# One weight split a tile, states beside their outputs, and one mask ahead of a fraction

## The chip, the core and the metric

The kernel runs on one core of a Trainium2 chip. Its engines are TensorE (PE, with its weight loads shown as PEld), VectorE (DVE), ScalarE (ACT), GpSimd (POOL) and the DMA queues, most of them fed by SyncE (SP). Each engine works through its own queue in order and waits on semaphores. The metric is the time of one execution in microseconds (us), lower is better.

## The reference, cut to what matters

```python
state = alpha[:, :, t, :, None] * state + einsum('bhd,bhe->bhde', k[:, :, t], v[:, :, t])   # for each of 768 t
y[:, :, t] = einsum('bhd,bhde->bhe', q[:, :, t], state)      # 4 batches, 8 heads, 48 x 48 states
...
x = y as (3072, 384)
h = x @ w_in; g = h * cos(h); x = g @ w_out                  # 384 -> 2048 -> 384
h = maximum(maximum(x @ w1, x @ w2), x @ w3); out = h @ w_out2   # 384 -> 768 -> 384
```

All in fp32. A decayed linear attention, then a cosine-gated layer, then a layer with a maximum of three products.

## The kernel before

**Precision.** A matrix product in fp32 is made of three in fp32r: each operand is split into a high part (a copy by ACT) and a low part (operand minus high part, by DVE or POOL), and `split_mm` issues high*high, low*high and high*low (L1293 to L1295).

**Stages.** The 768 steps of time are cut into 6 chunks of 128 tokens (x 4 batches = 512 columns). The attention of a chunk is 16 units (a pair of heads in one batch). The first layer's 2048 hidden features are 16 tiles of 128; in general, tile `i` of chunk `c` runs beside unit `i` of the attention of chunk `c + 1`. Chunk 0 has nobody to run beside, so its layer is cut in two half steps of 256 columns. The first half step, on which everything here turns, does tiles 0 to 15 for the first two batches while the units 8 to 15 of chunk 0 are still being done. Only units 0 to 7 stand ahead of it. The second half step (tiles counted on as 16 to 31) does the other two batches beside the attention of chunk 1.

**One tile of the first half step.** PE: `hidden1(i)` (9 matmuls into one of three banks in turn), then `accumulate1(i - 3)` (9 matmuls), then, for tiles in `SCORE_AT` (5 to 9, 11 to 13), `stage1` of a unit (scores and transposed keys), and, for tiles in `OUTPUT_AT` (6 to 9, 11 to 14), `outputs` and `increment` of the unit whose scores were made in a tile before. Units 8 to 15 alternate between two score banks: `stage1(0, u)` waits until the mask of unit `u - 1` is done and until the state of unit `u - 2` has been copied out of the bank. ACT: `turn(i)` (h in turns), `rounded(i)`, `g_high(i - 1)`, `cosines(i)`. DVE: `fraction(i)` between `rounded` and `cosines`, then `gate(i)`. POOL: `g_low(i)`, for which `accumulate1(i)` waits. So one tile's chain is hidden, turn, round, fraction, cosine, gate, high part, low part, accumulate.

**Other work laid between them by hand.** ACT also copies the high parts of the first layer's weights (`high_weights(k)`, one 128x768 copy a tile of weights, called "high k" below), the units' first states (`first_state(u)`, two 48x48 copies), splits of the keys and of x. The low parts of the weights (`low_weights(k)`, "low k") are made by DVE for k = 5, 8, 9, 10, 11 (table `low0`) and by POOL for the others (three pieces of 256 columns each). `hidden1(k)` waits for low k. DVE further does the masks of scores (`mask_scores`, waited for by `outputs`), the scan of the decays, its reciprocals (`inverse`), and POOL the products with the decays (`mul_decay`, `mul_inverse`). The order of each engine is what the program text says: there is no scheduler. `x_high0(3)` and `x_low0(3)`, in tile 15, split the last part of the second half step's x.

Of the kernel before, what the change touches and what calls it, by code (L numbers as in the profile page):

```python
# [17 lines left out]
UNITS = PAIRS * BATCH  # L18
TILES1 = FF1 // P
# [32 lines left out]
SCORE_AT = dict(zip((5, 6, 7, 8, 9, 11, 12, 13), range(FIRST_UNITS, UNITS)))  # L52
OUTPUT_AT = dict(zip((6, 7, 8, 9, 11, 12, 13, 14), range(FIRST_UNITS, UNITS)))
# [15 lines left out]
def build(nc, qka, val, wa, wb, spill, out):  # L69
# [8 lines left out]
    with ctx:  # L78
# [454 lines left out]
        def _(act):  # L533
# [20 lines left out]
            def high_weights(k):  # L554
                at = slice(k * W1COLS, (k + 1) * W1COLS)
                act.wait_ge(S[f"stage_in{k % SLOTS1}"], 16 * (k // SLOTS1 + 1))
                nc.scalar.activation(w_hi[:, at], stage[k % SLOTS1], ACT.Copy).then_inc(S["whi_done"], 1)

            def first_state(u):

                p, b = place0(u)
                act.wait_ge(S["inc_done"], u + 1)
                for row, col in ((0, 0), (64, HD)):
                    rr, cc = slice(row, row + HD), slice(col, col + HD)
                    nc.scalar.activation(state[rr, p * BATCH + b, cc], banks(u)[1][rr, cc],
                                         ACT.Copy).then_inc(S["state_done"], 1)
# [98 lines left out]
            for i in range(TILES1):  # L665
                last = i == TILES1 - 1
                if i == 10:
                    x_high0(2)
                if last:
                    x_high0(3)  # L670
                if i - 1 in OUTPUT_AT and not last:
                    first_state(OUTPUT_AT[i - 1])
                turn(i, True)
                if i == 1:
                    g_high(0, True)
                rounded(i)
                if i > 4:
                    g_high(i - 1, True)
                if i in (3, 8, 14):
                    split_keys(*{3: (0, 2), 8: (0, 3), 14: (1, 0)}[i])  # L680
                cosines(i, True)
                if 0 < i < 5:
                    high_weights(4 + i)
                if i in (1, 2, 3):
                    g_high(i, True)
                if 3 < i and 5 + i < TILES1:
                    high_weights(5 + i)
            g_high(TILES1 - 1, True)
            first_state(UNITS - 1)

            def split_high(t, s, part):

# [146 lines left out]
        def _(dve):  # L839
# [168 lines left out]
            ahead0 = {**{i: (0, 2, 2 + i) for i in range(2)}, **{i + 3: (0, 3, i) for i in range(4)},  # L1008
                      **{i + 8: (1, 0, i) for i in range(4)}, **{i + 13: (1, 1, i) for i in range(3)}}
            scan0 = {8: (1, 0), 10: (1, 1)}  # L1010
            low0 = {1: (5,), 5: (8,), 6: (9,), 7: (10, 11)}
            for i in range(TILES1):
                if i == 10:
                    x_low0(2)
                if i == TILES1 - 1:
                    x_low0(3)
                fraction(i, True)
                if i in scan0:
                    scan(*scan0[i])
                if i in SCORE_AT:  # L1020
                    mask_scores(0, SCORE_AT[i])
                early = i and i not in scan0 and i not in SCORE_AT
                if i in ahead0 and early:
                    inverse(*ahead0[i], ahead0[i][0] % 2)
                gate(i, True)
                if i == 2:
                    scan(0, 3)
                if i in ahead0 and not early:
                    inverse(*ahead0[i], ahead0[i][0] % 2)
                for k in low0.get(i, ()):  # L1030
                    low_weights(k)
# [523 lines left out]
```

## Time and profile before

| what | value |
|---|---|
| time, median of 3 runs | 842.2 us (842.09 to 842.33) |
| the profiled execution: its own time | 843.79 us |
| the profiled execution: its span, first to last instruction | 842.1 us |
| mean granted TensorE clock | 0.998 |
| PE busy in the span | 823.2 us (98%) |
| DVE, ACT, POOL busy | 582.0, 428.0, 245.7 us |
| first half step, from PE's first `hidden1` to the first of the next half step | 24.6 to 73.2 us of the span |

In the trace, times are counted from the span's start. A line of a timeline has start, duration, engine, line, operation, output and inputs, and in brackets how long the engine sat idle before it and for what. Matmuls overlap each other: what counts for PE is the distance from start to start. Also on ACT, DVE and POOL a successor's start lies some 0.1 us before the recorded end of the one ahead.

### The profile page before, as it was taken

The numbers are of one execution on the slowest core, as the hardware profiler recorded it, in microseconds if no ns is written. First come the engines' busy times: TensorE is split into PE (matmuls) and PEld (weight loads), VectorE is DVE, ScalarE is ACT, GpSimd is POOL, SyncE is SP. The second block draws the span as 40 slices with busy tenths as digits, with TensorE's granted clock in tenths as the row PEclk, the third lists the DMA queues.
The fourth block names the chain that finished last, engine by engine and source line by source line (L and its number), as shares of the span: only waits on it lengthen the run. The fifth ranks groups of instructions, "written<-read, shape, count | busy, mean of one in ns | idle before, by whom it ended". The sixth has DMA issues, their size and how long they took to land.

```text
span 842.1 us, 15514 instructions
## 1 busy us (share of the span) xinstructions
PE 823.2 (98%) x5446; PEld 757.6 (90%) x5446; DVE 582.0 (69%) x1080; ACT 428.0 (51%) x933; POOL 245.7 (29%) x272
## 2 busy tenths in 40 slices
PE   5899999999999999999999999999999999999998
PEld 5789998888888888888888888899999999999998
DVE  7797776877687767776874477676664655665554
ACT  4887775444554454445544456554343534334333
POOL 7886673444244425432442133200000000000000
PEclk9999999999999999999999999999999999999999
DMA  8832432322042204211312002210111010100001
GB/s 240 262 110 62 110 78 74 87 58 58 29 123 57 58 29 122 59 52 35 94 67 76 7 35 72 94 57 1 39 39 38 39 39 37 37 35 3 1 39 38
DMA packets 13778, 54.48 MB, mean 65 GB/s; under 512 B 1968, under 2 KB 2480, under 8 KB 13712
## 3 DMA queue, kind: packets, MB, share of 16 engines
q1 hardware_dynamic: 12992, 49.70, 20.6%
q0 software_dynamic: 720, 3.93, 1.2%
q8 instruction: 38, 0.62, 0.3%
q14 instruction: 28, 0.23, 0.1%
HBM read 44.19 MB, written 9.44 MB: 64 GB/s over the span
## 4 chain that ended last, share of the span: by engine, by line
PE 95%; DVE 2%; ACT 2%; issue 1%; ACTq 0%; DVEq 0%
PE h_ps L1293 7%; PE h_ps L1295 7%; PE h_ps L1294 7%; PE acc_pair L1293 5%; PE acc_pair L1294 5%; PE acc_pair L1295 5%; PE h_ps L1399 4%; PE score L1399 4%; PE h_ps L1401 4%; PE h_ps L1400 4%; PE score L1401 4%; PE score L1400 4%; PE acc_last L1293 3%; PE acc_last L1295 3%; PE acc_last L1294 3%; PE score L1257 3%
## 5 line engine op out<-in xcount | busy, mean ns | idle before, releaser
L463 POOL TENSOR_TENSOR work<-work 128x512 f32<-128x512 f32 (+1 forms) x90 | 119.5, 1328 | 278.8 <-DVE work L993 261.6
L635 ACT ACTIVATE work<-work 128x512 f32<-128x512 f32 (+1 forms) x112 | 63.7, 569 | 136.6 <-POOL work L463 123.0
L1293 PE MATMUL h_ps<-x_hi,w_hi 128*128 128x512 f32 (+1 forms) x282 | 111.3, 395 | 1.8 <-DVE x_lo L929 1.5
L979 DVE TENSOR_TENSOR work<-work,h_ps 128x512 f32<-128x512 f32 (+1 forms) x94 | 58.6, 623 | 67.3 <-ACT work L635 66.6
L1295 PE MATMUL h_ps<-x_lo,w_hi 128*128 128x512 f32 (+1 forms) x282 | 104.3, 370 | 0.0
L1294 PE MATMUL h_ps<-x_hi,w_lo 128*128 128x512 f32 (+1 forms) x282 | 103.5, 367 | 0.0
L871 DVE RECIPROCAL inv_decay<-decay 112x128 f32<-112x128 f32 x96 | 89.6, 942 | 0.5
L642 ACT ACTIVATE g_hi<-work 128x512 fp32r<-128x512 f32 (+1 forms) x112 | 63.5, 567 | 43.0 <-DVE work L979 41.7
L1293 PE MATMUL acc_pair<-g_hi,w_hi 128*128 128x512 f32 (+1 forms) x224 | 81.7, 365 | 0.1
L1295 PE MATMUL acc_pair<-g_lo,w_hi 128*128 128x512 f32 (+1 forms) x224 | 80.4, 359 | 0.0
L1294 PE MATMUL acc_pair<-g_hi,w_lo 128*128 128x512 f32 (+1 forms) x224 | 80.4, 359 | 0.0
L528 POOL DMA_DIRECT2D out<-raw x5 | 2.9, 575 | 258.9 <-DVE raw L1182 258.9
L985 DVE TENSOR_TENSOR g_lo<-work,g_hi 128x512 fp32r<-128x512 f32 x80 | 61.1, 764 | 14.9 <-ACT g_hi L642 13.6
L615 ACT ACTIVATE work<-h_ps 128x512 f32<-128x512 f32 (+1 forms) x83 | 46.8, 564 | 30.7 <-PE h_ps L1295 29.6
L1295 PEld LDWEIGHTS h_ps<-x_lo,w_hi 128*128 128x128 f32 x282 | 53.6, 190 | 9.6
L1293 PEld LDWEIGHTS h_ps<-x_hi,w_hi 128*128 128x128 f32 x282 | 53.9, 191 | 9.1 <-issue 1.8
L1399 PE MATMUL h_ps<-x_hi,w_hi 128*128 128x256 f32 x216 | 61.7, 286 | 0.0
L1399 PE MATMUL score<-x_hi,w_hi 128*128 128x256 f32 x216 | 61.7, 286 | 0.0
L1400 PE MATMUL score<-x_hi,w_lo 128*128 128x256 f32 x216 | 61.1, 283 | 0.0
L1400 PE MATMUL h_ps<-x_hi,w_lo 128*128 128x256 f32 x216 | 61.1, 283 | 0.0
L1401 PE MATMUL h_ps<-x_lo,w_hi 128*128 128x256 f32 x216 | 60.8, 282 | 0.0
L1401 PE MATMUL score<-x_lo,w_hi 128*128 128x256 f32 x216 | 60.8, 282 | 0.0
(232 smaller groups left out, 2402.2 us busy)
## 6 DMA issues: line engine op xcount, KB each, us to landing
v_all<-val SPq DMA_DIRECT2D x24, 576.0 KB, 3.7
raw<-qka SPq DMA_DIRECT2D x46, 291.0 KB, 4.6
block_out<-x SPq DMA_DIRECT2D x6, 768.0 KB, 6.0
x_in<-block_out SPq DMA_DIRECT2D x6, 768.0 KB, 4.3
raw<-wb SPq DMA_DIRECT2D x12, 384.0 KB, 3.2
out<-raw POOLq DMA_DIRECT2D x5, 768.0 KB, 3.5
stage_own<-wa SPq DMA_DIRECT2D x6, 384.0 KB, 7.7
x<-wa SPq DMA_DIRECT2D x6, 384.0 KB, 7.0
```

The lines of the kernel that those rows point to most:

```text
L463: nc.gpsimd.tensor_tensor(frac[:, cols], turns[:, cols], whole[:, cols], ALU.subtract).then_inc(S["frac_done"], 1)
L635: nc.scalar.activation(cosine[:, cols], frac[:, cols], ACT.Sin, scale=-TURN if half and t < POOL_FRAC else TURN).then_inc(S["cos_done"], 1)
L642: nc.scalar.activation(g_hi[:, odd, at], gated[:, cols], ACT.Copy).then_inc(S["ghi_done"], 1)
L871: nc.vector.reciprocal(inv_decay[R, s, b].rearrange("d (h n) -> d h n", h=2), decay[R, s, b].rearrange("d (h n) -> d h n", h=2)[:, :, D_LO ...
L979: nc.vector.tensor_tensor(gated[:, cols], cosine[:, cols], h, ALU.mult).then_inc(S["g_done"], 1)
L985: nc.vector.tensor_tensor(g_lo[:, odd, at], gated[:, cols], g_hi[:, odd, at].bitcast(fp32), ALU.subtract).then_inc(S["glo_done"], 1)
L1293: mm(ps, w_hi[:, w_at], xh, start=first, stop=False, skip_group_check=shared)
L1294: mm(ps, w_lo[:, w_at], xh, start=False, stop=False, skip_group_check=shared)
L1295: return mm(ps, w_hi[:, w_at], xl, start=False, stop=final, skip_group_check=shared)
L1399: mm(ps, hi, x_h, start=start, stop=False, skip_group_check=grown)
L1400: mm(ps, lo, x_h, start=False, stop=False, skip_group_check=grown)
L1401: return mm(ps, hi, x_l, start=False, stop=stop, skip_group_check=grown)
```

## The change

Three edits of the first half step, and no instruction is added or taken out.

1. ACT's `high_weights` stand one a tile: high 5 to 15 in tiles 1 to 11. Before, tile 4 had high 8 and high 9, and tiles 5 to 10 had high 10 to 15. High 9 to 15 thus move one tile later.
2. ACT's `first_state(u)` stands in the tile of the unit's outputs, behind `cosines(i)` and ahead of the weights; before, it stood at the head of the next tile (that of unit 15 at the end of the half step; it now stands in tile 14, ahead of `x_high0(3)`).
3. DVE: the mask of unit 8 stands ahead of `fraction(5)` and no longer behind it. Low 8 moves from tile 5 to 6, low 9 from 6 to 7, low 10 stays in 7, and low 11 moves from 7 to 9.

```diff
@@ ACT, loop over the tiles of the first half step
                 if last:
                     x_high0(3)
-                if i - 1 in OUTPUT_AT and not last:
-                    first_state(OUTPUT_AT[i - 1])
                 turn(i, True)
...
                 cosines(i, True)
-                if 0 < i < 5:
+                if i in OUTPUT_AT:
+                    first_state(OUTPUT_AT[i])
+                if 0 < i < TILES1 - 4:
                     high_weights(4 + i)
                 if i in (1, 2, 3):
                     g_high(i, True)
-                if 3 < i and 5 + i < TILES1:
-                    high_weights(5 + i)
             g_high(TILES1 - 1, True)
-            first_state(UNITS - 1)
@@ DVE, loop over the tiles of the first half step
-            low0 = {1: (5,), 5: (8,), 6: (9,), 7: (10, 11)}
+            low0 = {1: (5,), 6: (8,), 7: (9, 10), 9: (11,)}
...
+                if i == 5:
+                    mask_scores(0, SCORE_AT[i])
                 fraction(i, True)
                 if i in scan0:
                     scan(*scan0[i])
-                if i in SCORE_AT:
+                if i in SCORE_AT and i != 5:
                     mask_scores(0, SCORE_AT[i])
```

ACT in the tiles 4 (from its cosine) to 6. L557 is `high_weights`, L615 `turn`, L623 `rounded`, L642 `g_high`, L635 `cosines`, L565 `first_state`; x2 and x2_in are staging slots, high 8 and 9 come from x2, high 10 and 11 from x2_in. Before:

```order
L635 ACTIVATE work<-work 128x256
L557 ACTIVATE w_hi<-x2 128x768 x2
L615 ACTIVATE acc_last<-acc_last 128x256
L623 ACTIVATE work<-acc_last 128x256
L642 ACTIVATE g_hi<-work 128x256
L635 ACTIVATE work<-work 128x256
L557 ACTIVATE w_hi<-x2_in 128x768
L615 ACTIVATE h_ps0<-h_ps0 128x256
L623 ACTIVATE work<-h_ps0 128x256
L642 ACTIVATE g_hi<-work 128x256
L635 ACTIVATE work<-work 128x256
L557 ACTIVATE w_hi<-x2_in 128x768
```

The same place after:

```order
L635 ACTIVATE work<-work 128x256
L557 ACTIVATE w_hi<-x2 128x768
L615 ACTIVATE acc_last<-acc_last 128x256
L623 ACTIVATE work<-acc_last 128x256
L642 ACTIVATE g_hi<-work 128x256
L635 ACTIVATE work<-work 128x256
L557 ACTIVATE w_hi<-x2 128x768
L615 ACTIVATE h_ps0<-h_ps0 128x256
L623 ACTIVATE work<-h_ps0 128x256
L642 ACTIVATE g_hi<-work 128x256
L635 ACTIVATE work<-work 128x256
L565 ACTIVATE state<-score0 48x48 x2
```

One copy of weights (high 9) has moved behind tile 5's cosine, high 10 behind tile 6's, and the state of unit 8 stands straight behind tile 6's cosine.

DVE from `gate(4)` on. Before, L1002 is `fraction`, L892 `mask_scores`, L979 `gate`, L871 `inverse`, L940 `low_weights`, L861 `scan` (each number is 3 less in the changed file). Before, tiles 4 to 6:

```order
L979 TENSOR_TENSOR work<-work,h_ps1 128x256
L1002 SCALAR_TENSOR_TENSOR work<-work,acc_last 128x256
L892 TENSOR_TENSOR scores<-score0,mask 128x304
L979 TENSOR_TENSOR work<-work,acc_last 128x256
L871 RECIPROCAL inv_decay<-decay 112x128
L940 TENSOR_TENSOR w_lo<-x2,w_hi 128x768
L1002 SCALAR_TENSOR_TENSOR work<-work,h_ps0 128x256
L892 TENSOR_TENSOR scores<-score1,mask 128x304
L979 TENSOR_TENSOR work<-work,h_ps0 128x256
L871 RECIPROCAL inv_decay<-decay 112x128
```

The same place after:

```order
L976 TENSOR_TENSOR work<-work,h_ps1 128x256
L889 TENSOR_TENSOR scores<-score0,mask 128x304
L999 SCALAR_TENSOR_TENSOR work<-work,acc_last 128x256
L976 TENSOR_TENSOR work<-work,acc_last 128x256
L868 RECIPROCAL inv_decay<-decay 112x128
L999 SCALAR_TENSOR_TENSOR work<-work,h_ps0 128x256
L889 TENSOR_TENSOR scores<-score1,mask 128x304
L976 TENSOR_TENSOR work<-work,h_ps0 128x256
L868 RECIPROCAL inv_decay<-decay 112x128
L881 COPY from_mid<-decay 112x2x2
L937 TENSOR_TENSOR w_lo<-x2,w_hi 128x768
```

The first mask has passed the fraction, and low 8 stands behind the reciprocal of tile 6 and no longer behind that of tile 5.

DVE once more, in the changed kernel, from the scan of tile 8 to the next scan, in tile 10:

```order
L858 SCALAR_TENSOR_TENSOR decay<-raw,starts 112x528
L889 TENSOR_TENSOR scores<-score1,mask 128x304
L976 TENSOR_TENSOR work<-work,acc_last 128x256
L868 RECIPROCAL inv_decay<-decay 112x128
L999 SCALAR_TENSOR_TENSOR work<-work,h_ps0 128x256
L889 TENSOR_TENSOR scores<-score0,mask 128x304
L976 TENSOR_TENSOR work<-work,h_ps0 128x256
L868 RECIPROCAL inv_decay<-decay 112x128
L937 TENSOR_TENSOR w_lo<-x2_in,w_hi 128x768
L921 TENSOR_TENSOR x_lo0<-y_ps,x_hi 96x2x256
L999 SCALAR_TENSOR_TENSOR work<-work,h_ps1 128x256
L858 SCALAR_TENSOR_TENSOR decay<-raw,starts 112x528
```

Low 11 (L937) is what is new in this stretch, at the end of tile 9.

## Rows read from the trace of the kernel before

**Rows 1.** Busy of PE, PEld, DVE, ACT, POOL by stretch; clock, DMA share, GB/s.

```profile
40.00:80.00 40.00, 36.93 (x320) 36.10 (x318) 33.15 (x63) 32.01 (x88) 29.02 (x38) 1.00 0.33 91
80.00:842.00 762.00, 757.81 (x4940) 694.49 (x4938) 517.34 (x962) 370.68 (x786) 185.57 (x184) 1.00 0.18 53
```

**Rows 2.** Waits of PE, 38 to 70 us, longest: total, times, longest one.

```profile
PE y_ps L1272 <- DVE scores L892: 1.9, 1, 1.9
```

**Rows 3.** Timeline of PE: hidden or accumulate of tiles, scores, outputs.

```profile
42.62 0.43 PE L1272 MATMUL y_ps<-scores,v_all 128*96 128x128 f32 x2 [1.93 <-DVE scores L892]
...
46.65 0.46 PE L1257 MATMUL score<-q_dec,k_split 112*128 112x128 f32 x2 [1.07 <-ACT state L565]
...
47.75 0.36 PE L1293 MATMUL acc_last<-x_hi,w_hi 128*128 128x256 f32 x1
...
56.73 0.28 PE L1293 MATMUL acc_last<-x_hi,w_hi 128*128 128x256 f32 x1
...
61.06 0.28 PE L1293 MATMUL acc_pair<-g_hi,w_hi 128*128 128x256 f32 x1
...
62.02 0.28 PE L1295 MATMUL acc_pair<-g_lo,w_hi 128*128 128x256 f32 x1
62.37 0.46 PE L1257 MATMUL score<-q_dec,k_split 112*128 112x128 f32 x2
...
74.38 0.28 PE L1293 MATMUL acc_pair<-g_hi,w_hi 128*128 128x256 f32 x1
...
75.61 0.46 PE L1257 MATMUL score<-q_dec,k_split 112*128 112x128 f32 x2
```

**Rows 4.** Timeline of ACT: tiles 4, 5, 6, the key split of 8, and 15.

```profile
39.39 1.56 ACT L557 ACTIVATE w_hi<-x 128x768 fp32r<-128x768 f32 x2
40.86 0.36 ACT L615 ACTIVATE acc_last<-acc_last 128x256 f32<-128x256 f32 x1
...
42.13 0.42 ACT L635 ACTIVATE work<-work 128x256 f32<-128x256 f32 x1 [0.18 <-DVE work L1002]
42.45 0.83 ACT L557 ACTIVATE w_hi<-x_in 128x768 fp32r<-128x768 f32 x1
...
46.09 0.42 ACT L565 ACTIVATE state<-score 48x48 f32<-48x48 f32 x2
...
50.50 1.25 ACT L589 ACTIVATE k_split<-k_dec 64x512 f32<-64x512 f32 x2
```

**Rows 5.** Timeline of DVE: tiles 4 to 8, and the scan of tile 10.

```profile
39.81 0.36 DVE L979 TENSOR_TENSOR work<-work,h_ps 128x256 f32<-128x256 f32 x1
...
42.01 0.47 DVE L892 TENSOR_TENSOR scores<-score,mask 128x304 f32<-128x304 f32 x1
...
45.82 0.95 DVE L871 RECIPROCAL inv_decay<-decay 112x128 f32<-112x128 f32 x1
...
46.70 0.95 DVE L940 TENSOR_TENSOR w_lo<-x,w_hi 128x768 fp32r<-128x768 f32 x1
...
48.80 2.38 DVE L940 TENSOR_TENSOR w_lo<-x_in,w_hi 128x768 fp32r<-128x768 f32 x2
...
51.43 1.46 DVE L861 TENSOR_TENSOR_SCAN decay<-raw,starts 112x528 f32<-112x528 f32 x1
...
57.89 2.10 DVE L861 TENSOR_TENSOR_SCAN decay<-raw,starts 112x528 f32<-112x528 f32 x1
```

**Rows 6.** Timeline of POOL: low weights, low parts of g (g_lo), tiles 7 to 14.

```profile
50.68 1.10 POOL L471 TENSOR_TENSOR g_lo<-work,g_hi 128x256 fp32r<-128x256 f32 x1 [0.32 <-ACT g_hi L642]
51.73 3.06 POOL L453 TENSOR_TENSOR w_lo<-stage_own,w_hi 128x256 fp32r<-128x256 f32 x3
...
55.45 2.14 POOL L453 TENSOR_TENSOR w_lo<-stage_own,w_hi 128x256 fp32r<-128x256 f32 x3
...
58.83 1.69 POOL L471 TENSOR_TENSOR g_lo<-work,g_hi 128x256 fp32r<-128x256 f32 x1
...
73.42 0.73 POOL L471 TENSOR_TENSOR g_lo<-work,g_hi 128x256 fp32r<-128x256 f32 x1 [3.44 <-ACT g_hi L642]
```

## The prediction, made before the changed kernel was run

> **What bounds the kernel now.** I read the busy time by stretch first. Behind 80 us PE is busy for 757.81 of 762.00 us at full granted clock, with DVE at 517 and ACT at 371 [rows 1]: from there on the time is PE's own work, so what PE gains or loses ahead of that point arrives at the end unchanged. Of the 40 us before it PE is busy for 36.93: 3.07 us are missing [rows 1]. The view of PE's waits, read next, says where: 1.9 us for the mask of unit 8 [rows 2]. PE's timeline has it as the gap that ends at 42.62, and beside it one of 1.07 that ends at 46.65, for the state of unit 8 [rows 3]: together 3.0. Nothing else of that size exists, so 3.1 us (0.4%) is about the most that this change can give. Whether it gives them depends on the chains of ACT, DVE and POOL, read last.
>
> **Part 1: the two waits.** Both come from tile 4's double weight copy. The two copies start at 39.39 and the turn of tile 5 at 40.86 [rows 4], so a copy costs 0.73 from start to start. From a turn to the cosine, through round and fraction, it is 42.13 - 40.86 = 1.27, and from the cosine to the next instruction 0.32 [rows 4]. A pair of states takes 0.44 (0.42 and the usual distance).
> With one copy, turn 5 starts at 40.12, cosine 5 at 41.39, high 9 at 41.71, turn 6 at 42.44, cosine 6 at 43.71, the state of unit 8 at 44.03. The score that waits for this state started 46.65 - 46.09 = 0.56 behind it [rows 3, 4], so now 44.6.
> The mask: gate 4 ends at 39.81 + 0.36 = 40.17 [rows 5] and is touched by nothing in the change, the mask follows at 40.2, and the output came 42.62 - 42.01 = 0.61 behind it [rows 3, 5]: 40.8, in place of 42.62. ACT and DVE are both free for this, and the unit's scores are older. The fraction that the mask now precedes waits for ACT until 40.9, so the mask's 0.47 costs nothing there.
> Then PE does tile 7's hidden and waits for accumulate 4 (its g_lo stands behind POOL's old work, about 0.3), then for the score at 44.6, and has its output of unit 9 done at 45.7, where before the next hidden started at 47.75 [rows 3]. So far 2.05 us are won.
>
> **Part 2: low 8 becomes late.** Hidden 8 needs low 8, which has moved behind the reciprocal of tile 6. Gate 6 starts when cosine 6 has ended (0.42 [rows 4]), at 44.15, the reciprocal at 44.5. From reciprocal to low weights it is 46.70 - 45.82 = 0.88, and the subtraction takes 0.95 [rows 5]: low 8 runs from 45.36 to 46.3. Hidden 8 starts at 46.4 and not at 45.7. Of 2.05 us 1.35 are left.
>
> **Part 3: the stretch of tiles 7 to 11.** Fraction 7 stands behind low 8 (46.2), so cosine 7 is at 46.65. Add 0.32, the states 0.44, high 11 0.73: turn 8 at 48.15. Turn, round and g_hi take 1.0 until the key split, which takes 1.28 (two of 1.25 together [rows 4]): cosine 8 at 50.4, states, high 12 at 51.2, turn 9 at 51.9, so ACT's tile 9 could have its cosine at 53.2.
> DVE does low 9 and low 10 from 47.4. A pair took 2.38, where one alone takes 0.95: the POOL subtraction beside it took 1.10 in place of 0.73 [rows 5, 6]. These are two engines blocking each other, and I take the pair's time: fraction 8 at 49.8. The scan of tile 8 took 1.46 with the same kind of neighbour [rows 5]; mask 11 is at 51.6, gate 8 at 51.9, then reciprocal (0.33 + 0.87), fraction 9 at 53.1, cosine 9 at 53.6, state 0.44, high 13 from 54.35 to 55.2. Gate 9 follows at 54.05, the reciprocal, and low 11 from 55.25 to 56.2. Hidden 11 waits for it: 56.3, in place of 56.73 [rows 3]. Left: 0.4 us.
>
> **Part 4: POOL, the term that decides.** Before, POOL worked without a break from 51.73 (low 12) to 58.83 + 1.69 = 60.52 (g_lo of tile 9) [rows 6], and accumulate 9 started at 61.06 [rows 3]: a margin of 0.5 us only. Now low 13 cannot start before high 13 is there, at 55.2, where before it started at 55.45 [rows 6], right behind its predecessor. From there POOL has the three pieces (2.14 - 0.05), two products with decays (58.83 - 55.45 - 2.1 = 1.3) and the g_lo (0.73), 4.1 us. On top come the blocks. The scan of tile 10 cost the g_lo of tile 9 1.69 - 0.73 = 0.96 before; it does so again, since it moves to about 57.1 and into POOL's busy stretch. New is low 11, which starts at 55.25 beside low 13: a block of 0.4 (the g_lo at 50.68) to 0.96: 1.10 and 1.69 against 0.73 [rows 6]. Low 12 gained the like (3.06 before for what takes 2.14 [rows 6]), but that gain is lost, as POOL waits for high 13. Together 55.2 + 4.1 + 1.9 = 61.2; with 0.4 for low 11 it is 60.7. I take the upper one, as two instructions start within 0.1 us of each other and the whole subtraction lies in the way. Accumulate 9 then starts at 61.25, 0.2 later than before.
> On what this block is: the row shows a POOL subtraction stretched from 0.73 to 1.69 beside a DVE scan [rows 5, 6]. The Trainium skill (SBUF — State Buffer, section Who interferes with whom) says that a DVE instruction with two SBUF inputs and a GpSimd instruction that reads SBUF exclude each other for a whole instruction. The trace agrees. By that rule the block of low 11 is 0.95 less what has already run, so the sum would be the 61.2 above; by the mildest row it would be 60.7.
>
> **Part 5: what remains.** The score of tile 12 had a gap ahead of it: it starts 0.35 behind the previous matmul, where 0.12 is usual (62.02, 62.37) [rows 3]. It waited for a state copied at the head of tile 12, which now comes in tile 11, at 61.3 or earlier: -0.2. In tile 14, the states of unit 15 now stand ahead of x_high0(3), so g_hi 14 and with it g_lo 14 come 0.44 later against PE. The g_lo ends at 73.42 + 0.73 = 74.15 and accumulate 14 starts at 74.38 [rows 3, 6], margin 0.2: +0.25. The score at 75.61 waited for that same state (its 0.46 in place of 0.39 shows a restart), and no longer does: -0.2. The start of the second half step on x_low0(3) has some 0.7 us to spare. DMA: the loads of weights behind low 8 and low 9 are issued up to 1.7 us later, and are used more than 5 us behind that: nothing.
>
> **Sum.** +0.2 (accumulate 9) + 0.1 (restart) - 0.2 + 0.25 - 0.2 = +0.15 us against the span of 842.1, so 842.25. The profiled execution took 843.79 in all, 1.7 above its span, but the median of the plain runs is 842.2; the difference is carried over to that: 842.35, and I write 842.3. A measurement of this kernel can tell 0.2% (1.7 us) from no change; the forecast is no change.
>
> **Rivals.**
> *The gain survives (chance 0.30).* If low 9 and 10 take 1.7 in place of 2.38, high 13 and low 11 come 0.5 earlier, POOL is less blocked and accumulate 9 starts at 60.6 or before. Then part 2's and 3's rests stay: 0.5 to 1.2 us, so 841.4. For it: one DVE subtraction beside a POOL one took 0.95 only [rows 5]. Against: the pair of the very same shape took 2.38.
> *The two waits go and nothing takes their place (0.05).* 3.1 us less the 0.25 above and some bubble: 840.0 or up to 840.5. Against it stand two due times, low 8 at 46.3 and low 11 at 56.2, that follow from rows of DVE without any block.
> *Slower: low 11 loses the port (0.15).* If POOL's first piece of low 13 starts ahead of low 11, and the second too, low 11 ends at 57.3: hidden 11 starts 0.6 later than before, POOL's chain is pushed as well, and part 5 is added: 843.0. It decides once low 11 ends behind 56.6. The scan at 57.89 that took 2.10 and not 1.46 [rows 5] shows that DVE can lose twice.
> *The forecast (0.50).* Two waits of 3.0 us go, and waits for low 8, low 11, g_lo 9 and g_lo 14 come in their place.
>
> **Range and chances.** The forecast alone spans 841.9 to 842.7 (the block of low 11 between 0.4 and 0.96). With the surviving gain down to 841.2, and the slower case up to 842.9, at most 2 in 10 are left out. Faster by over 0.2% needs the case without new waits: 0.05. Slower by over 0.2% would need three lost turns in a row: 0.03. Within 0.2%: 0.92.
>
> **What would show it.** Right: the output at 40.8 and the score at 44.6 in PE's timeline; a wait of PE for low weights of DVE ahead of hidden 8 (0.7) and ahead of hidden 11; a wait for POOL's g_lo at accumulate 9; low 13 of POOL starting with an idle gap for ACT. Wrong: PE running without a gap from 46 to 61 (then the gain stays), or accumulate 9 with a margin; low 9 and low 10 in under 1.9 together; any new wait behind 80 us, of which this reckoning has none.

## The result and the profile after

The changed kernel takes 846.78 us (median of 5 runs, 844.61 to 847.26). The kernel before, run beside it, takes 842.2 (842.09 to 842.78). The ratio is 1.0047, with a 95% interval of 1.0032 to 1.0062: slower by about 4 us (the two medians are 4.6 apart), where I had forecast no change and a range of 841.2 to 842.9.

The profiled execution of the changed kernel took 845.47 us in all, with a span of 843.8. Busy time by stretch (PE, PEld, DVE, ACT, POOL, each with its count; clock, DMA share, GB/s), the rows that answer to [rows 1]:

```profile
40.00:80.00 40.00, 34.70 (x292) 33.44 (x293) 34.17 (x59) 29.70 (x80) 27.21 (x35) 1.00 0.33 90
80.00:842.00 762.00, 759.66 (x4960) 696.63 (x4958) 518.90 (x963) 372.34 (x791) 186.57 (x186) 1.00 0.17 53
```

PE lacks 5.3 us of the 40 where it lacked 3.07 before [rows 1]; behind 80 us it is as dense as ever. So the loss lies where the change was made. This execution has only a part of it: from the cosine of tile 4 to the end of its span it takes 843.8 - 38.4 = 805.4 us, and the kernel before 842.1 - 39.1 = 803.0. The other part is worked out at the end of the experiments. The waits of PE from 22 to 90 us (total, times, longest one) answer to [rows 2]:

```profile
PE score L1256 <- ACT state L565: 2.6, 2, 2.2
PE h_ps L1292 <- DVE x_lo L926: 1.5, 1, 1.5
PE acc_last L1292 <- DVE w_lo L937: 1.4, 2, 0.8
PE acc_pair L1292 <- POOL g_lo L471: 1.2, 2, 0.9
```

The 1.9 for the mask is gone. The forecast waits are there: low weights of DVE (1.4), g_lo (1.2), a short one for a state (0.4). One is in no step of the prediction: 2.2 us for a state. PE's timeline, answering to [rows 3], has it at 67.74, ahead of the score of tile 13:

```profile
43.91 0.46 PE L1256 MATMUL score<-q_dec,k_split 112*128 112x128 f32 x2 [0.43 <-ACT state L565]
...
45.78 0.36 PE L1292 MATMUL acc_last<-x_hi,w_hi 128*128 128x256 f32 x1 [0.56 <-DVE w_lo L937]
...
55.51 0.36 PE L1292 MATMUL acc_last<-x_hi,w_hi 128*128 128x256 f32 x1 [0.84 <-DVE w_lo L937]
...
61.00 0.38 PE L1292 MATMUL acc_pair<-g_hi,w_hi 128*128 128x256 f32 x1 [0.94 <-POOL g_lo L471]
...
67.74 0.46 PE L1256 MATMUL score<-q_dec,k_split 112*128 112x128 f32 x2 [2.16 <-ACT state L565]
```

The whole trace lies 0.7 us earlier than that of before (cosine 4 at 38.36 and not 39.07). That is no work of the change: in the traces of all kernels below, whose program is the same up to there, this cosine lies anywhere from 37.60 to 39.10. So 0.7 must be added to compare with rows of before.

Who held the state? ACT's timeline: it waited 4.88 us for DVE's fraction of tile 12, and copied the state of unit 13 behind its cosine.

```profile
66.86 0.42 ACT L635 ACTIVATE work<-work 128x256 f32<-128x256 f32 x1 [4.88 <-DVE work L999]
67.18 0.42 ACT L565 ACTIVATE state<-score 48x48 f32<-48x48 f32 x2
```

And DVE's timeline, answering to [rows 5]:

```profile
61.08 0.42 DVE L976 TENSOR_TENSOR work<-work,acc_last 128x256 f32<-128x256 f32 x1 [1.49 <-POOL g_lo L471]
61.42 0.94 DVE L868 RECIPROCAL inv_decay<-decay 112x128 f32<-112x128 f32 x1
62.28 3.53 DVE L874 TENSOR_TENSOR to_mid<-decay,from_mid 112x4 f32<-112x4 f32 x1
65.74 0.76 DVE L881 COPY from_mid<-decay 112x4 f32<-112x4 f32 x1
66.42 0.41 DVE L999 SCALAR_TENSOR_TENSOR work<-work,h_ps 128x256 f32<-128x256 f32 x1
```

A product of four columns took 3.53 us, and the copy of four columns behind it 0.76. In the kernel before the same two, which I call the pair, took

```profile
63.13 0.54 DVE L877 TENSOR_TENSOR to_mid<-decay,from_mid 112x4 f32<-112x4 f32 x1
63.59 0.16 DVE L884 COPY from_mid<-decay 112x4 f32<-112x4 f32 x1
```

POOL's timeline of the changed kernel, answering to [rows 6]:

```profile
60.22 1.43 POOL L471 TENSOR_TENSOR g_lo<-work,g_hi 128x256 fp32r<-128x256 f32 x2
61.60 2.12 POOL L453 TENSOR_TENSOR w_lo<-x,w_hi 128x256 fp32r<-128x256 f32 x3
63.67 0.73 POOL L471 TENSOR_TENSOR g_lo<-work,g_hi 128x256 fp32r<-128x256 f32 x1
64.37 2.11 POOL L453 TENSOR_TENSOR w_lo<-x,w_hi 128x256 fp32r<-128x256 f32 x3
```

POOL's subtractions run back to back at their undisturbed 0.7 us while the product is pending, and end at about 62.3, 63.0, 63.7, 64.4, 65.1 and 65.8. The product was issued at 62.28 and ended with the last of these: DVE let four or five ends pass. Before, it got in as soon as the subtraction that was running had ended (63.13 to 63.67).

### The profile page after: what moved, and what is told of

Read it like the earlier page. It is cut to its first block, busy times and chain, and to the rows that moved or that the text cites. A ratio compares the mean times of both kernels' runs of the same rounds, so it can differ in the third digit from the quotient of the medians.

```text
span 843.8 us, 15514 instructions
## 1 busy us (share of the span) xinstructions
PE 821.8 (97%) x5446; PEld 755.3 (90%) x5446; DVE 585.4 (69%) x1080; ACT 427.7 (51%) x933; POOL 245.5 (29%) x272
## 4 chain that ended last, share of the span: by engine, by line
PE 91%; ACT 2%; DVE 2%; issue 2%; POOL 2%; DMA 0%; ACTq 0%; POOLq 0%; DVEq 0%
PE h_ps L1292 7%; PE h_ps L1294 6%; PE h_ps L1293 6%; PE acc_pair L1292 5%; PE acc_pair L1293 5%; PE acc_pair L1294 5%; PE h_ps L1398 4%; PE score L1398 4%; PE h_ps L1400 4%; PE h_ps L1399 4%; PE score L1400 4%; PE score L1399 4%; PE acc_last L1292 3%; PE acc_last L1293 3%; PE acc_last L1294 3%; PE y_ps L1275 2%
## 5 line engine op out<-in xcount | busy, mean ns | idle before, releaser
L635 ACT ACTIVATE work<-work 128x512 f32<-128x512 f32 (+1 forms) x112 | 63.7, 569 | 139.8 <-POOL work L463 122.9
L642 ACT ACTIVATE g_hi<-work 128x512 fp32r<-128x512 f32 (+1 forms) x112 | 63.5, 567 | 42.7 <-DVE work L976 41.4
L615 ACT ACTIVATE work<-h_ps 128x512 f32<-128x512 f32 (+1 forms) x83 | 46.7, 562 | 30.8 <-PE h_ps L1294 29.7
```

Source lines behind the costliest of these rows:

```text
L635: nc.scalar.activation(cosine[:, cols], frac[:, cols], ACT.Sin, scale=-TURN if half and t < POOL_FRAC else TURN).then_inc(S["cos_done"], 1)
L642: nc.scalar.activation(g_hi[:, odd, at], gated[:, cols], ACT.Copy).then_inc(S["ghi_done"], 1)
```

## The experiments

Seventeen kernels ran. Each is compared with runs of the kernel before on the same chip, whose median was between 842.55 and 843.11. "Changed" and "before" say which kernel an edit starts from.

**Is the pair the loss?** First, in the changed kernel, a reciprocal of one input from SBUF in place of the product. This leaves the product out in tile 11, so the output is another and only the time is read:

```diff
+ if a == 1 and p == 0:
+     dve.wait_ge(S["inv_done"], BATCH * g + BATCH)
+     nc.vector.reciprocal(to_mid[R, s], inv_decay[R, s, :, HALF - 1])
+ else:
      nc.vector.tensor_tensor(to_mid[R, s], decay[R, s, :, HALF], from_mid[R, 1 - odd, p], ALU.mult)
```

> The changed kernel, but in tile 11 the product for to_mid (112x4, two inputs in SBUF, 3.53 us in the trace after) is a reciprocal of one input: the product is left out there, so the output differs and only the time is read. Theory A (this tiny instruction loses the shared SBUF port to POOL's unbroken run of subtractions again and again; all the rest is as forecast): 842.3 +- 0.4 us, with runs within 0.7 us of each other, and the tile's instructions take under 0.3 us. Rival B (the loss is the late high weights and POOL's chain to g_lo 9, and to_mid only shows it): stays at 844.5 to 847.

Measured 844.64 (844.17 to 849.67, 11 runs), ratio 1.0031 [1.0020, 1.0043]. A miss, and a telling one. DVE's timeline:

```profile
61.77 0.18 DVE L876 RECIPROCAL to_mid<-inv_decay 112x4 f32<-112x4 f32 x1
61.86 3.26 DVE L885 COPY from_mid<-decay 112x4 f32<-112x4 f32 x1
```

The one-input reciprocal got in at once (0.18), and the stall moved to the copy. So a second input from SBUF is not needed for it. Next the pair as a whole goes to tile 15, in the changed kernel and in the kernel before:

```diff
-                if b == BATCH - 1:
+                if b == BATCH - 1 and not (a == 1 and p == 0):
...
+                if i == TILES1 - 1:
+                    middle(1, 0, 1)          # product and copy
```

> The changed kernel with the whole computation, but the two tiny instructions behind the last reciprocal of that group (product to_mid and copy from_mid) moved from tile 11 to tile 15, where POOL is idle. Theory A: 842.3 +- 0.4 us with a narrow spread, and the product takes 0.1 us. Rival B: 844.5 to 847 as before.

> The kernel before, with only the tiny product and copy moved from tile 11 to tile 15 (whole computation). In the trace of before they took 0.54 and 0.16 us in tile 11, DVE was not what PE waited for there. Theory A (in before the pair got in at the first gap, by the phase of POOL's stream): 842.3 +- 0.4, no change. Rival C (before too loses to POOL in some executions, which its median hides): lower median by up to 0.5 and a narrower spread than the 841.9 to 843.7 of before.

The changed kernel without the pair in tile 11 takes 842.97 (842.62 to 844.23, 11 runs), ratio 1.0005 [0.9996, 1.0014]. Its product takes 0.10 and its copy 0.15, and PE's waits from 38 to 90 us are

```profile
PE acc_last L1300 <- DVE w_lo L943: 1.4, 2, 0.9
PE acc_pair L1300 <- POOL g_lo L471: 1.2, 2, 0.9
PE score L1264 <- ACT state L565: 0.4, 1, 0.4
```

These are the waits of the forecast: 3.0 us in place of 3.0 us. The kernel before with the same edit takes 843.05 (ratio 1.0005 [0.9996, 1.0014]): it lost nothing by the pair. So the pair's place in the changed schedule is the whole loss of 4 us, and the rest of the change is worth nothing that these runs can tell.

**Which half of the change brings it?** ACT's part alone (the diff's edits 1 and 2) and DVE's part alone (edit 3):

```diff
# ACT alone: in the changed kernel, DVE as before (the mask of unit 8 too, left out here)
-            low0 = {1: (5,), 6: (8,), 7: (9, 10), 9: (11,)}
+            low0 = {1: (5,), 5: (8,), 6: (9,), 7: (10, 11)}
# DVE alone: in the changed kernel, ACT as before (the states too, left out here)
-                if 0 < i < TILES1 - 4:
+                if 0 < i < 5:
                     high_weights(4 + i)
+                if 3 < i and 5 + i < TILES1:
+                    high_weights(5 + i)
```

> The kernel before with ACT's part of the change alone (one weight a tile, states in the tile of their outputs); DVE's order is that of before. High 13 is late for POOL as in the changed kernel, so POOL runs unbroken up to tile 11's tiny product. Theory A: slower with a wide spread, 843 to 847, if the product lies in POOL's unbroken run in its trace, with over 1 us for it. Rival B: 844 to 847 with a short product. If neither: low 11 in tile 7 waits for high 11 and costs DVE about 0.8 us, 842.5.

> The kernel before with DVE's part alone (mask of unit 8 ahead of the fraction of tile 5, low 8, 9 and 11 later); ACT's order is that of before, so high 12 and 13 are early for POOL. Theory A: the time goes by whether the tiny product meets an unbroken POOL: 841.5 to 842.5 and narrow if it takes under 0.7 us, up to 846 if not. Rival B (late high weights are the loss): 841.2 to 842.3, whatever the product takes.

ACT's part alone: 845.69 (845.3 to 846.0, 5 runs), ratio 1.0035 [1.0022, 1.0048]. DVE's part alone: 846.11 (845.75 to 846.4), ratio 1.004 [1.0027, 1.0053]. Either half brings the stall, on the copy in the one (3.54 us) and on the product in the other (3.53).

```profile
60.73 0.77 DVE L874 TENSOR_TENSOR to_mid<-decay,from_mid 112x4 f32<-112x4 f32 x1
61.42 3.54 DVE L881 COPY from_mid<-decay 112x4 f32<-112x4 f32 x1
```

Those two rows are of ACT's part alone. The moved mask by itself, from the kernel before (`mask_scores` of tile 5 ahead of `fraction(5)`, nothing else):

> The kernel before with only the mask of unit 8 moved ahead of the fraction of tile 5. By the steps of the prediction fraction 5 does not wait for the mask, and the output of unit 8 comes about 0.7 us earlier (fraction 5 starts at 41.7 as before, the mask at 40.2 in its idle time): PE then waits longer for the state of unit 8 at 46.65 (0.4 earlier), so 0.3 to 0.6 us are gained if nothing else moves: 841.9. Theory A: if the tiny product meets POOL's unbroken run in its trace with 3 us, it is 844 to 846 instead, in spite of the smaller wait.

843.29 (843.05 to 843.54), ratio 1.0008 [0.9999, 1.0017]; expected was a gain. PE's longest wait shows why there is little: the 1.9 for the mask became a longer one for the state, which ACT still copied in the next tile. PE waits 2.5 us in place of 3.0, and that half us doesn't show in the time.

```profile
PE score L1259 <- ACT state L565: 2.5, 1, 2.5
```

**Does the rest of the forecast leave something to win?** The pair in tile 15, and low 8 and low 11 ahead of their reciprocals:

```diff
+                if i in (6, 9):
+                    for k in low0.get(i, ()):
+                        low_weights(k)
```

> The changed kernel with product and copy in tile 15 (as in the run at 842.97) and, besides, low 8 and low 11 ahead of the reciprocals of tiles 6 and 9. Whole computation. By the prediction's own steps the waits of PE for low 8 (0.8) and low 11 (0.8 in the trace) go; PE then waits for g_lo 9 until about the same time as now, since POOL's chain hangs on high 13. So if POOL's chain is what bounds (prediction, part 4), the gain over the run at 842.97 is 0 to 0.4 us: 842.6 to 843.0. If low 8 and low 11 were what binds, it is 0.8 or more: 842.1 or less.

842.9 (842.42 to 844.03), ratio 1.0006 [0.9997, 1.0015]. PE's wait for DVE's low weights fell from 1.4 to 0.9 (that for low 8 is gone, that for low 11 stays) and the one for g_lo from 1.2 to 1.0; no time clear of the noise came of it. Which chain bounds next isn't shown, and no version beat the kernel before.

**Why does DVE lose so many turns?** Two probes put a test stretch behind the whole kernel before: POOL subtracts 128x256 blocks without a pause, and DVE issues tiny products and copies between reciprocals; in the second, at 28 positions against POOL's instruction, twice over for the products and twice for the copies, once each beside a POOL that waits for a semaphore after every third subtraction. PE and ACT have nothing to do in these stretches, unlike in the kernel.

```diff
+            for n in range(96):                       # POOL
+                last = piece_of(n)
+            for n in range(28):                       # DVE
+                filler(96 + 4 * n)                    # a reciprocal of growing width
+                nc.vector.tensor_tensor(to, decay[R, 0, :, HALF], from_mid[R, 0, 0], ALU.mult)
```

> The kernel before, with a test stretch behind its end that measures the disputed cost by itself: POOL runs 150 subtractions 128x256 back to back, beside it DVE runs reciprocals 112x128 with, between them, 10 tiny products (112x4, two SBUF inputs), 10 tiny copies (112x4) and 4 subtractions 128x384; then POOL runs bursts of three with a pause, beside 9 more tiny products. Theory A: in the unbroken stream some or all tiny products and copies take 2.8 to 3.6 us (four or five POOL instructions), the reciprocals 0.94 throughout, and in the bursts no product takes over 1.5 us. Rival D (a tiny instruction waits for the POOL instruction that runs, and gets in at its end): none takes over 0.8 us, and the 3.5 us of the changed kernel have another cause.

> The kernel before with another test stretch behind its end. In the first probe all tiny instructions waited 0.5 us, but each arrived at the same point of POOL's instruction, since the last wait had set the phase. Now the reciprocal ahead of each has another width (96 to 204 columns), so that 28 tiny products and then 28 tiny copies arrive at points spread over POOL's 0.69 us; each once beside a stream of POOL without semaphores and once beside one in groups of three with a semaphore, as its low weights are. Theory E (a tiny instruction that arrives in the last few hundredths of a us of a POOL instruction loses several turns in a row): most take 0.1 to 0.8 us, and one or two of each sweep 2.8 to 3.6. Rival D (it always gets in at the next end of a POOL instruction): all under 0.8. Rival F (a stream in which POOL's next instruction waits for nothing never lets go for 3 us): over 2.8 us at all phases beside the first stream and not beside the second.

The first gave 0.50 to 0.59 for every tiny instruction, the second these (duration min/median/max in ns):

```profile
L1278 DVE TENSOR_TENSOR v_all<-decay,from_mid x56: 91/336/627, 848.6 to 948.8; 112x4 f32<-112x4 f32 x56
L1280 DVE COPY v_all<-decay x56: 98/344/633, 979.8 to 1080.1; 112x4 f32<-112x4 f32 x56
```

None waited longer than one POOL subtraction takes. So neither a long unbroken stream of POOL nor the phase of the request is enough by itself. The phase was then tried in the real place, by a reciprocal of 48 or 60 columns ahead of the pair:

```diff
+                        if a == 1 and p == 0:
+                            nc.vector.reciprocal(idle[R, 0:48], decay[R, s, 0, 1:49])   # 60 in the kernel before
```

> The changed kernel with one reciprocal of 48 columns (0.36 us, one input) ahead of the product for to_mid in tile 11, so that it arrives in the middle of a POOL instruction and not 0.02 us ahead of its end. Theory E (phase): the product takes under 0.8 us, time 842.5 to 843.5. Rival G (any place in that stretch of POOL loses until the third piece of low 15): the product still takes 3.1 us, time 844.5 to 847.

> The kernel before with one reciprocal of 60 columns (0.44 us) ahead of the product for to_mid in tile 11, so that it arrives 0.04 us ahead of the end of a POOL instruction instead of 0.48. Theory E (phase): the product or the copy takes about 3 us, time 844 to 846. Rival G: in at the next end, 0.1 to 0.8 us, time 842.5 to 843.

The changed kernel stays at 847.26 (846.51 to 847.66), ratio 1.0054 [1.0037, 1.0070], with a product of 3.21 us; the kernel before stays at 843.09, ratio 1.0001 [0.9991, 1.0011], with a product of 0.15. The phase is out.

**Is it POOL's semaphores?** My next theory, H in the expectations, was that DVE gets in where a wait of POOL was met shortly before. In the kernel before, the g_hi for which POOL's g_lo of tile 11 waits ended at 63.34, just ahead of the end at which DVE got in. So I gave the changed kernel a wait at that place that is met just as shortly before, and as its control the same wait met long before; and I let the kernel before go on, behind low 14, with low 15, whose inputs are long there.

```diff
# fresh wait: + 1; old wait: + 0 (changed kernel, ahead of g_low(11))
+                if i == 11:
+                    pool.wait_ge(S["inc_done"], OUTPUT_AT[i] + 1)
# kernel before: low 15 ahead of g_low(11)
+                if i == 10:
+                    pool.wait_ge(S["scan_done"], 6)
+                    low_weights(15)
```

> Changed kernel; GpSimd waits in addition for the state product of unit 12 ahead of g_low of tile 11 (profiled: that product starts at 63.03 and takes 0.39, GpSimd comes to the place at 63.67, so the wait is met about 0.25 us before and costs nothing). H (the vector engine gets in only where a wait of GpSimd was met shortly before it came to it, as g_high 11 was in the kernel before, at 63.34 for 63.61): the tiny product gets in at 63.7, takes about 1.3 us instead of 3.53, the score's wait for the state falls from 2.2 to nearly none, 842.3 to 843.2. G (what counts is the stretch of low weights itself, whatever is waited for): still 3.2 to 3.6 us, 845 to 847.5.

> The same wait at the same place, but for the state product of unit 11, over some 4 us before. H: nothing changes against the changed kernel, 3.2 to 3.6 us for the tiny product, 844.5 to 847.5. If instead one more instruction in GpSimd's queue is enough to let the vector engine in (I): as with the fresh wait, 842.3 to 843.2. G: 845 to 847.5.

> Kernel before; low weights of tile 15 are split right behind those of tile 14, ahead of g_low of tile 11, so that at 63.61, where the vector engine got in, GpSimd now goes on with a piece whose inputs and waits were all met over 4 us before. H: the tiny product issued at 63.13 now stalls, 2.8 us or more, as in the changed kernel, and the kernel loses its 2 to 4 us: 844.5 to 847. G' (it is the rest of the changed schedule, not GpSimd's waits): still 0.54 us; accumulate 11 comes up to 2.1 us later, since g_low 11 does, of which some 0.5 to 1.5 shows: 842.7 to 844.

847.59 (ratio 1.0051 [1.0037, 1.0064]) with the fresh wait, 847.62 (1.0047 [1.0033, 1.0061]) with the old one, both with a product of 3.53 to 3.54 us. The kernel before with low 15 in front: 843.4, ratio 1.0001 [0.9992, 1.0010], and the product got in as soon as the piece that was running had ended, though the next one waits for nothing:

```profile
60.38 4.19 POOL L453 TENSOR_TENSOR w_lo<-x,w_hi 128x256 fp32r<-128x256 f32 x6
...
61.98 0.52 DVE L880 TENSOR_TENSOR to_mid<-decay,from_mid 112x4 f32<-112x4 f32 x1
62.42 0.16 DVE L887 COPY from_mid<-decay 112x4 f32<-112x4 f32 x1
```

My theory H fell on both sides. The changed kernel with POOL made to wait for the pair, between two pieces of low 14:

```diff
+                    low_weights(14, (0,))
+                    pool.wait_ge(S["mid_done"], 5)
+                    low_weights(14, (1, 2))
```

> Changed kernel; GpSimd waits for the tiny product and copy between the first and the second piece of the low weights of tile 14 (about 62.3 us, when the reciprocal ahead of them ends). The cause being that the tiny pair loses the port turn after turn: the product takes under 0.3 us, the copy too, GpSimd idles 0.2 to 0.4 us, and the loss is gone, 842.3 to 843.2, as where the pair came in tile 15 (842.97). If the tiny pair only shows a wait that has another cause (the product's data): it stays over 2.8 us and GpSimd waits with it, 846 to 849.

843.52 (842.67 to 844.6, 11 runs), ratio 1.0004 [0.9995, 1.0013]. The loss is gone for a pause of 0.19 us:

```profile
62.76 0.10 DVE L878 TENSOR_TENSOR to_mid<-decay,from_mid 112x4 f32<-112x4 f32 x1
62.78 0.16 DVE L885 COPY from_mid<-decay 112x4 f32<-112x4 f32 x1
...
63.02 1.43 POOL L453 TENSOR_TENSOR w_lo<-x,w_hi 128x256 fp32r<-128x256 f32 x2 [0.19 <-DVE from_mid L885]
```

**A pause of POOL.** One mark told the short cases, as far as the pair stood in its old place and POOL did not wait for it, from the stalls: in the kernel before, and in its variants with the mask, the delay and low 15 in front, POOL sits idle for 0.31 us ahead of the g_lo of tile 10, some 2 us before the pair is issued; here is the row of before.

```profile
60.84 0.74 POOL L471 TENSOR_TENSOR g_lo<-work,g_hi 128x256 fp32r<-128x256 f32 x1 [0.31 <-ACT g_hi L642]
```

In every kernel with a stall its last idle time had ended 10 us or more before (at 51.60 in the changed kernel). So the last two kernels put that pause into the changed kernel, and were to take it out of the kernel before.

```diff
# changed kernel, a pause ahead of g_low(10)
+                if i == 10:
+                    pool.wait_ge(S["turns_done"], 13)
# kernel before, meant to have no pause: low 14 ahead of g_low(10), low 15 ahead of g_low(11)
+                if i == 10:
+                    low_weights(14)
+                if i == 11:
+                    pool.wait_ge(S["scan_done"], 6)
+                    low_weights(15)
                 g_low(i)
```

> Changed kernel; GpSimd waits ahead of g_low of tile 10 for the turns of tile 12 (ScalarE, ready at about 61.25; GpSimd comes there at 60.9), so that it idles some 0.3 us there, as it does at that place in the kernel before and in all runs in which the tiny pair took under 1 us, and in none in which it stalled. J (the pair is held off only where GpSimd has run for a long time without a pause; an idle time of 0.3 us some 2 us ahead is enough): the product takes 0.5 us or less, 842.3 to 843.5. K (the pause is a mark of the other schedule and does nothing): 3.2 to 3.6 us, 844.5 to 848.

> Kernel before; low weights of tile 14 go ahead of g_low of tile 10, and those of tile 15 ahead of g_low of tile 11, so that GpSimd has no idle time from 50.7 until the tiny product is issued at 63.1. J: the product or the copy now takes 2.8 us or more, and the time is 844.5 to 848. K: under 1 us for both; the later g_low (1.7 to 2 us) delays accumulate 10 and 11, 842.5 to 845; the verdict is from the duration of the pair.

With the pause the changed kernel takes 843.85 (843.25 to 844.31, 11 runs), ratio 1.0010 [1.0001, 1.0019]. POOL's idle time and the pair:

```profile
62.02 0.74 POOL L471 TENSOR_TENSOR g_lo<-work,g_hi 128x256 fp32r<-128x256 f32 x1 [0.38 <-ACT h_ps L617]
...
62.11 0.95 DVE L870 RECIPROCAL inv_decay<-decay 112x128 f32<-112x128 f32 x1
62.97 0.49 DVE L876 TENSOR_TENSOR to_mid<-decay,from_mid 112x4 f32<-112x4 f32 x1
63.39 0.16 DVE L883 COPY from_mid<-decay 112x4 f32<-112x4 f32 x1
```

A pause that ends 0.95 us ahead of the request, and about 3 of the 4 us are back. The kernel before with low 14 and low 15 moved ahead takes 846.9 (846.27 to 847.23), ratio 1.0046 [1.0033, 1.0060], the loss of the changed kernel, but at another instruction than I had expected: the scan of tile 10, 4.19 us where it took 2.10 [rows 5]. Four instructions of POOL that had been issued after it (a product with decays, g_lo 9, two pieces of low 14) went first, and the pair came that much later.

```profile
56.97 4.19 DVE L866 TENSOR_TENSOR_SCAN decay<-raw,starts 112x528 f32<-112x528 f32 x1
...
64.29 0.50 DVE L882 TENSOR_TENSOR to_mid<-decay,from_mid 112x4 f32<-112x4 f32 x1
```

The scan's median in the kernel before is 1.25 us (24 times), so it waited 2.9 us. The pair's product took 0.50, again 2.3 us behind an idle time of POOL (0.31, ended at 61.99): the pause had moved with the rest and was not gone. This run settles one half and spoils the other: it shows a second instruction that a change in POOL's order alone makes lose several turns, but what was changed in POOL's stream lay behind the scan's request, not ahead of it. The last pause ahead of it is the same in both kernels, some 7 us back. So "a pause shortly before" describes all cases in which DVE got in quickly near one, and doesn't explain why the scan of before waited 0.85 us and this one 2.9, nor why the product of ACT's part alone, above, got in at the next end (0.77) with no pause for 9 us.

**Why 4 us, when PE waits 2.2 longer?** The granted clock gives the rest. Here is the stretch behind PE's wait in the profiled execution of the changed kernel (PE, PEld, DVE, ACT, POOL; clock, DMA share, GB/s):

```profile
68.00:72.00 4.00, 4.00 (x38) 4.00 (x38) 3.08 (x6) 3.16 (x10) 1.37 (x2) 1.00 0.73 149
```

And here in the changed kernel with the old wait, whose product (3.54) and whose wait of PE (2.16, to 68.01) are the same:

```profile
68.00:72.00 4.00, 3.99 (x22) 4.00 (x23) 2.09 (x4) 1.81 (x7) 0.84 (x2) 0.57 0.68 149
```

PE had stood idle for 2.16 us. Half a us after it had started again the clock fell to 0.50 (1.2 of 2.4 GHz) and was back at 1.00 from 72 us on: 22 matmuls in place of 38, though PE had started only 0.3 us later. From the cosine of tile 4 to the end, this execution takes 845.9 - 38.6 = 807.3 us and the one with the fresh wait 845.9 - 39.0 = 806.9, against 805.4 without the low stretch and 803.0 in the kernel before. The version with the pair in tile 15 takes 841.5 - 38.1, about 803.5. So the stall itself costs about 1.9 us and the clock behind it 1.5 to 1.9 more. Of the eight traces with a stall, six have that low stretch: both halves of the change, the delay, the fresh and the old wait, and the kernel before with low 14 and low 15 moved ahead. The two without it are the profiled execution of the changed kernel and the run with the reciprocal, where PE's pause was 1.48 us and the median 2.1 us above that of the kernel before. None of the other traces has it there.

## Why the prediction was wrong

**Parts 1 to 3 held.** With 0.7 added: the output of unit 8 at 40.7 (forecast 40.8), the score at 44.6 (44.6), hidden 8 at 46.5 (46.4), hidden 11 at 56.2 (56.3). The steps in between fit too: low 8 ran from 44.69 + 0.7 = 45.4 (45.36), and low 9 and low 10 took 2.3 together (2.38).

**Part 4 held in kind and was too small.** Accumulate 9 came at 61.0 + 0.7 = 61.7, with the wait of 0.94 for g_lo; forecast was 61.25. The term was +0.2 and measured +0.64. The sign "low 13 of POOL starting with an idle gap for ACT" did not come. POOL waited for ACT ahead of low 12, and low 13 stood behind the g_lo of tile 8:

```profile
51.60 2.13 POOL L453 TENSOR_TENSOR w_lo<-stage_own,w_hi 128x256 fp32r<-128x256 f32 x3 [1.85 <-ACT w_hi L557]
53.67 2.28 POOL L471 TENSOR_TENSOR g_lo<-work,g_hi 128x256 fp32r<-128x256 f32 x1
55.91 3.06 POOL L453 TENSOR_TENSOR w_lo<-stage_own,w_hi 128x256 fp32r<-128x256 f32 x3
```

That g_lo took 2.28 in place of 0.73, and ended when these two instructions of DVE had:

```profile
54.47 0.89 DVE L937 TENSOR_TENSOR w_lo<-x_in,w_hi 128x768 fp32r<-128x768 f32 x1
55.28 0.67 DVE L921 TENSOR_TENSOR x_lo<-y_ps,x_hi 96x512 fp32r<-96x512 f32 x1
```

So the block of low 11, put at 0.4 to 0.96 on low 13, was 1.55 on the g_lo ahead of it, as x_lo followed low 11 at once. The scan's block was 0.95 (the middle piece of low 13 took 1.68), as forecast, but g_lo 9 was not the one to bear it.

**Part 5.** The score of tile 12 starts at 62.17, without the gap of before, as the term of -0.2 has it. In the version with the pair moved away accumulate 14 has a gap of 0.14 ahead of it (term +0.25), and nothing else that the profile lists stands behind 68 us. Together with part 4 the sum of +0.15 came out about right: that version takes about 803.5 us from the cosine of tile 4 to the end, against 803.0, and its ratio is 1.0005.

**The step that failed** is in part 5 and in the sum: they go from the score of tile 12 to tile 14 and put the score of tile 13 at nothing, without a reason. It needs the state of unit 13, which ACT copies in tile 12 behind a cosine, and that cosine needs DVE's fraction of tile 12. I did not follow what DVE has in its queue between gate 11 and that fraction: reciprocal, product, copy. The pair stood in the trace of before with 0.54 and 0.16 us, and no step costed it. The runs showed 3.53 and 0.76 us for it; ACT waited 4.88 us and PE 2.16. A second term stood at nothing: the prediction has PE at full clock throughout, and behind the pause of PE six of the eight traces with a stall have a stretch at 1.2 GHz, which cost 1.5 to 1.9 us.

**The slower rival had the right mechanism and the wrong size.** It had DVE lose the port twice, at low 11, 843.0, chance 0.15. Low 11 lost nothing (0.89 us). I wrote "Slower by over 0.2% would need three lost turns in a row: 0.03". It was four or five, and on an instruction of four columns, and the clock came on top. The Trainium skill (SBUF — State Buffer, section Who interferes with whom) has the loser blocked for whole instructions of the other engine, which the rows above agree with; it gives no bound on how many. The same section counts a copy among the instructions that can, under conditions on its operands, take the shared pair with a single input, and a one-input instruction outside those modes not; the runs agree: the copy took 3.26 and 3.54 us where the reciprocal of as many columns took 0.18. Its rule that the order of issue decides who blocks they don't bear out: the pending product was passed by four subtractions issued after it (and a fifth, issued 0.02 us after it), and the measurement decides.

**What stays open.** Why DVE is let in at the next end in one stretch of POOL and only after four or five in another. Shown: the cause is POOL's pending work (a wait of POOL for the pair ends it; so does a pause of 0.38 us), not the product's two inputs, the phase of the request, a wait met shortly before, or an unbroken stream alone. Not shown: what in the engine counts the turns, why 96 subtractions in a row let DVE in every time in the probe (there PE and ACT stood idle; whether that matters was not tried), and why the clock fell behind the same pause in most traces and not in all. The changed kernel's five runs spread over 844.6 to 847.3, which is about what the low stretch and a shift of the start could make; only one of the five has a trace, so which of them had it is not known.

## What to carry to other kernels

When a schedule is made tighter, list each small instruction on the engine that shares a port with a busy neighbour, and ask who waits behind it: its price is not its size but the neighbour's instructions that pass first, here up to five. And a pause of the engine at the bound can cost more than its length: 2 us of waiting became about 4 where PE's clock fell behind it. An idle gap of 0.3 us in the neighbour's stream can be worth keeping; where there is none, a wait of the neighbour for the small instruction costs 0.2 us and removed a loss of 4. A mask or a state that arrives earlier is worth nothing until its successor in the chain does too (the mask alone: 843.29).

## What the runs showed of the hardware

- A DVE instruction of 112x4 beside a stream of POOL subtractions (0.7 us each) took 3.2 to 3.5 us in seven kernels, 0.1 to 0.8 in others, and at most 0.63 in 112 trials of a synthetic stretch.
- The one-input copy of 112x4 is held off as well (3.26 and 3.54 us, against 0.15 with the port free), a one-input reciprocal of that size is not (0.18).
- The loser need not be the one that asks last. POOL's pieces kept their 0.72 to 0.74 us each while the product, issued before four of them, waited.
- A POOL subtraction waits for several DVE instructions too: the g_lo of tile 8 took 2.28 in place of 0.73, over low 11 and x_lo.
- A scan of 1.25 us (median) took 4.19 when only POOL's order behind it had been changed.
- Behind a pause of PE of 2.0 to 2.2 us the granted clock fell to 0.50 in six of seven traces, shortly after PE had started again, and cost 1.5 to 1.9 us more; behind the pause of 1.9 us for the mask it did so in one of seven, and behind one of 2.5 (the moved mask alone) not.
